# GpSimd writes the last 64 mixed columns twice; a pair of tiles leaves PSUM by one copy and one subtraction

## The reference: what is computed

```python
w = exp(weight_gen - max(weight_gen, axis=-1))       # (4, 4096, 8 heads, 7 taps)
w = w / (sum(w, axis=-1) + 1e-9)
# causal window of 7 rows, each head (24 columns) with its own weights
mix = einsum('bshk,bskhg->bshg', w, x_unfolded)       # (16384, 192)
h = mix @ w_in                                        # 192 -> 2048
g = where(h > 0, h, exp(min(h, 0)) - 1)
out = g @ w_out                                       # 2048 -> 192
```

## Time and profile before

| | |
|---|---|
| median of three runs | 1265.78 us |
| span of the profiled execution, first to last instruction | 1264.7 us |
| PE busy | 1207.9 us, 96% |
| PEld busy | 1088.5 us, 86% |
| ACT busy | 966.0 us, 76% |
| DVE busy | 822.4 us, 65% |
| POOL busy | 704.2 us, 56% |
| instruction fetches, queue 14 | 74 packets, 0.61 MB |
| instruction fetches, queue 8 | 10 packets, 0.16 MB |

### The profile page before, as it was taken

One profiled execution on the slowest core, in us unless ns is written; L12 is line 12 of the kernel. 1 busy time (PEld: TensorE's weight loads), 2 busy tenths in 40 slices (PEclk: granted clock), 3 DMA queues, 4 the chain that ended last, 5 costly groups with the idle time before them and its releaser, 6 DMA issues.

```text
span 1264.7 us, 21620 instructions
## 1 busy us (share of the span) xinstructions
PE 1207.9 (96%) x6848; PEld 1088.5 (86%) x6848; DVE 822.4 (65%) x1453; ACT 966.0 (76%) x1897; POOL 704.2 (56%) x298
## 2 busy tenths in 40 slices
PE   2799999999999999999999999999999999999998
PEld 2699998989899898998989989898998989989998
DVE  7866666666566666666666566666666666666665
ACT  3588878778788787787778787787777877877886
POOL 8666654556645466554566545566454665545600
PEclk9899999999999999999999999999999999999999
DMA  7011011111011110011110011110111100110000
GB/s 223 32 48 49 14 36 47 47 48 47 1 47 47 48 47 31 18 47 48 47 48 20 28 47 47 48 47 1 47 47 48 47 21 27 47 48 13 13 14 13
DMA packets 17124, 52.13 MB, mean 41 GB/s; under 512 B 1944, under 2 KB 8212, under 8 KB 17040
## 3 DMA queue, kind: packets, MB, share of 16 engines
q1 hardware_dynamic: 17040, 51.36, 12.0%
HBM read 38.77 MB, written 12.58 MB: 41 GB/s over the span
## 4 chain that ended last, share of the span: by engine, by line
PE 88%; issue 5%; DVE 4%; ACT 3%; DMA 0%; SPq 0%; ACTq 0%; POOL 0%; DVEq 0%; POOLq 0%
PE slot L593 44%; PE acc L599 27%; PE acc L603 15%; ACT em L425 1%; DVE wout L503 1%; PE slot L581 1%; DVE g_lo L554 1%; ACT em L431 1%; DVE slot L548 1%; ACT g_hi L438 1%; PE slot L583 1%; DVE prod L471 0%; DVE prod L475 0%; DMA xwin<-in_x_dram 0%; SPq L242 0%
## 5 line engine op out<-in xcount | busy, mean ns | idle before, releaser
L548 DVE SCALAR_TENSOR_TENSOR slot<-em,slot 128x512 f32<-128x512 f32 x512 | 356.4, 696 | 419.2 <-ACT em L431 417.6
L599 PE MATMUL acc<-wout,g_hi 128*128 128x384 f32 x2048 | 469.7, 342 | 29.0 <-DVE g_lo L554 29.0
L425 ACT ACTIVATE em<-slot 128x512 f32<-128x512 f32 x512 | 305.4, 597 | 232.7 <-PE slot L593 183.8
L599 PEld LDWEIGHTS acc<-wout,g_hi 128*128 128x128 f32 x2048 | 369.2, 188 | 71.0 <-DVE g_lo L554 26.1
L554 DVE TENSOR_TENSOR g_lo<-slot,g_hi 128x512 fp32r<-128x512 f32 x511 | 350.1, 685 | 1.9
L431 ACT ACTIVATE em<-em 128x512 f32<-128x512 f32 x512 | 323.5, 632 | 16.3
L603 PE MATMUL acc<-wout,g_lo 128*128 128x192 f32 x2048 | 327.0, 266 | 0.9 <-DVE g_lo L554 0.9
L603 PEld LDWEIGHTS acc<-wout,g_lo 128*128 128x128 f32 x2048 | 312.0, 190 | 3.2 <-DVE g_lo L554 1.2
L331 POOL TENSOR_TENSOR prod<-xwin,probs 128x5376 f32<-128x5376 f32 (+1 forms) x32 | 308.1, 9628 | 8.1 <-POOL probs L317 6.5
L438 ACT ACTIVATE g_hi<-slot 128x512 fp32r<-128x512 f32 x511 | 298.1, 583 | 12.8 <-DVE slot L548 11.3
L593 PE MATMUL slot<-xt,win_hi 128*128 128x512 f32 x512 | 214.9, 420 | 2.7 <-DVE xt L516 2.7
(11 more groups left out here) (47 smaller groups left out, 585.1 us busy)
## 6 DMA issues: line engine op xcount, KB each, us to landing
xwin<-in_x_dram SPq DMA_DIRECT2D x30, 960.0 KB, 4.7
out_dram<-outs SPq DMA_DIRECT2D x32, 384.0 KB, 2.4
wg<-in_weight_gen_dram SPq DMA_DIRECT2D x32, 112.0 KB, 2.3
wout_raw<-in_moe_w_out_dram SPq DMA_DIRECT2D x4, 384.0 KB, 9.5
win_raw<-in_moe_w_in_dram SPq DMA_DIRECT2D x1, 768.0 KB, 6.5
win_rest_raw<-in_moe_w_in_dram SPq DMA_DIRECT2D x2, 384.0 KB, 8.6
xwin<-in_x_dram SPq DMA_DIRECT2D x1, 768.0 KB, 11.0
xwin<-in_x_dram SPq DMA_DIRECT2D x1, 384.0 KB, 3.7
```

Of the source, the lines that this page charges most:

```text
L425: nc.scalar.activation(em[:, i % 2, :], slot[s][:], ACT.Exp).then_inc(s_exp, 1)
L548: nc.vector.scalar_tensor_tensor(out=slot[s][:], in0=em[:, i % 2, :], scalar=0.0, in1=slot[s][:], op0=ALU.min, op1=ALU.max).then_inc(s_g, 1)
L599: pe.matmul(acc[j][:, 0:2 * d_model], g_hi[:, f % GBUFS, chunk(j)], wout[:, f, :], start=(f == 0), stop=False)
```

## The change

GpSimd (and VectorE in the first block) writes each tile's last 64 columns twice side by side, so `mixed_rest` has 128 columns for each tile. TensorE transposes each tile's rest by itself, two transposes where there was one, and the slot is filled with 512 columns; both halves of the partitions hold the same 64 columns. ScalarE copies the whole slot at once to hi, and VectorE makes lo of it by one subtraction. The split of the weights moves into one array: `win_rest` has hi of w_in's last 64 rows on partitions 0 to 63 and lo on 64 to 127, so the subtraction that makes lo runs on 64 partitions. The five matmuls of the first product stay five: the two for the rest are now (hi; lo) of the weights with hi of x, and (hi; lo) with lo of x.

```diff
--- before.py
+++ after.py
@@ -72,7 +72,7 @@
-    XPARTS = 3
+    XPARTS = 1
@@ -121,8 +121,7 @@
-        win_rest_hi = sb("win_rest_hi", [P, d_ff], F32R)
-        win_rest_lo = sb("win_rest_lo", [P, d_ff], F32R)
+        win_rest = sb("win_rest", [P, d_ff], F32R)
@@ -135,10 +134,10 @@
-        mixed_rest = sb("mixed_rest", [P, 2, TILES, REST])
+        mixed_rest = sb("mixed_rest", [P, 2, TILES, 2, REST])
...
-        xt_lo = sb("xt_lo", [P, 2, N], F32R)
+        xt_lo = sb("xt_lo", [P, 2, 2, N], F32R)
@@ -224,6 +223,10 @@
+        def twice(t, tiles):
+
+            return t[:, :, P:].unsqueeze(2).broadcast_to([P, tiles, 2, REST])
+
@@ -307,8 +310,10 @@
-                    nc.gpsimd.tensor_tensor(win_rest_lo[:, cols], win_rest_raw[:, cols],
-                                            win_rest_hi[:, cols].bitcast(F32), ALU.subtract).then_inc(s_plo, 1)
+                    pool.wait_ge(s_psoft, b.count(SOFTMAX, 1))
+                    nc.gpsimd.tensor_tensor(win_rest[REST:, cols], win_rest_raw[REST:, cols],
+                                            win_rest[REST:, cols].bitcast(F32), ALU.subtract).then_inc(s_plo, 1)
+                    pool.wait_ge(s_plo, 1)
@@ -345,8 +350,8 @@
-                nc.gpsimd.tensor_tensor(mixed_rest[:, q, first_tile:, :], one[:, :, P:], two[:, :, P:],
-                                        ALU.add).then_inc(s_add, 1)
+                nc.gpsimd.tensor_tensor(mixed_rest[:, q, first_tile:, :, :], twice(one, TILES - first_tile),
+                                        twice(two, TILES - first_tile), ALU.add).then_inc(s_add, 1)
@@ -383,16 +388,13 @@
-                nc.scalar.activation(xt[:, parity, 0, k * W:(k + 1) * W], slot[s][:, 0:W], ACT.Copy).then_inc(s_xhi, 1)
-                for t in range(PAIR):
-                    half_of = slice(t * REST, (t + 1) * REST)
-                    nc.scalar.activation(xt[half_of, parity, 1, k * W + t * P:k * W + (t + 1) * P],
-                                         slot[s][half_of, W:W + P], ACT.Copy).then_inc(s_xhi, 1)
+                nc.scalar.activation(xt[:, parity, :, k * W:(k + 1) * W],
+                                     slot[s][:].rearrange("p (a c) -> p a c", a=2), ACT.Copy).then_inc(s_xhi, 1)
...
-                parts = ((win_hi, win_raw), (win_rest_hi, win_rest_raw))
+                parts = ((win_hi, win_raw), (win_rest, win_rest_raw))
@@ -484,7 +486,7 @@
-                    nc.vector.tensor_tensor(mixed_rest[:, q, 0:tiles, :], one_t[:, :, P:], two_t[:, :, P:],
+                    nc.vector.tensor_tensor(mixed_rest[:, q, 0:tiles, :, :], twice(one_t, tiles), twice(two_t, tiles),
@@ -492,10 +494,12 @@
-            for k, (lo, raw, hi) in enumerate(((win_lo, win_raw, win_hi), (win_rest_lo, win_rest_raw, win_rest_hi))):
-                dve.wait_ge(s_whi, 1 + k)
-                nc.vector.tensor_tensor(lo[:, cols], raw[:, cols], hi[:, cols].bitcast(F32),
-                                        ALU.subtract).then_inc(s_wlo, 1)
+            dve.wait_ge(s_whi, 1)
+            nc.vector.tensor_tensor(win_lo[:, cols], win_raw[:, cols], win_hi[:, cols].bitcast(F32),
+                                    ALU.subtract).then_inc(s_wlo, 1)
+            dve.wait_ge(s_whi, 2)
+            nc.vector.tensor_tensor(win_rest[REST:, cols], win_rest_raw[REST:, cols],
+                                    win_rest[REST:, cols].bitcast(F32), ALU.subtract).then_inc(s_wlo, 1)
@@ -507,15 +511,8 @@
-                nc.vector.tensor_tensor(xt_lo[:, parity, cols], slot[s][:, 0:W], xt[:, parity, 0, cols].bitcast(F32),
-                                        ALU.subtract).then_inc(s_xlo, 1)
-
-                for t in range(PAIR):
-                    half_of, other = (slice(a * REST, (a + 1) * REST) for a in (t, 1 - t))
-                    cols = slice(k * W + t * P, k * W + (t + 1) * P)
-                    nc.vector.tensor_tensor(xt[other, parity, 1, cols], slot[s][half_of, W:W + P],
-                                            xt[half_of, parity, 1, cols].bitcast(F32),
-                                            ALU.subtract).then_inc(s_xlo, 1)
+                nc.vector.tensor_tensor(xt_lo[:, parity, :, cols], slot[s][:].rearrange("p (a c) -> p a c", a=2),
+                                        xt[:, parity, :, cols].bitcast(F32), ALU.subtract).then_inc(s_xlo, 1)
@@ -579,8 +576,9 @@
-                rest = mixed_rest[:, parity, k * PAIR:(k + 1) * PAIR, :].rearrange("p t c -> p (t c)")
-                last = pe.transpose(slot[s][:, W:W + P], rest, ident[:])
+                for t in range(PAIR):
+                    rest = mixed_rest[:, parity, k * PAIR + t, :, :].rearrange("p a c -> p (a c)")
+                    last = pe.transpose(slot[s][:, W + t * P:W + (t + 1) * P], rest, ident[:])
@@ -588,8 +586,8 @@
-                        (win_hi[:, cols], xt_lo[:, parity, :]), (win_rest_hi[:, cols], xt[:, parity, 1, :]),
-                        (win_rest_lo[:, cols], xt[:, parity, 1, :]))):
+                        (win_hi[:, cols], xt_lo[:, parity, 0, :]), (win_rest[:, cols], xt[:, parity, 1, :]),
+                        (win_rest[:, cols], xt_lo[:, parity, 1, :]))):
```

## The result

The changed kernel takes 1247.99 us (median of 4 runs, 1247.65 to 1248.53), before 1265.85 us. The ratio is 0.986, with a 95% interval from 0.9836 to 0.9884.

A forecast was written before the change was run, and what follows sets the result against it. TensorE, busy 1207.9 of 1264.7 us, was taken as the bound, with waits behind ScalarE's loop branch. 1265.8 + 7.1 (transposes) + 0 - 20.5 (waits gone) = 1252.4 us, range 1250 to 1257.

The forecast's parts named there:

- The branch: At ScalarE's loop branch: missing instructions delay g_lo for TensorE; the shorter program removes all 13 waits, -20.5 us.
- the pieces: ScalarE's program is fetched 128 instructions at a time; its loop needs four such parts in place of five.
- the second silence: ScalarE's 2.04 us stop right behind the loop's first instruction; it goes whether three or four pieces are held.
- Which of three or four pieces is held: ScalarE's instruction memory: with four nothing is fetched in the loop; with three one stop of 1.96 us remains.
- The rival that the silences stay: ScalarE still fetches two pieces in a row at each of 13 branches; transposes cost alone, 1272.9 us; chance 0.12.
- the other rule of size: Trainium skill's window, two blocks of 256 instructions: a loop over a border fetches at every branch, before and after.
- the 13 waits of the list: TensorE's waits for g_lo behind the branch, 1.58 us each, 20.5 us together, all expected to go.
- The transposes: On TensorE, one more for each pair, 62 outside the fill, up to 0.115 us each: +7.1 us.
- Copies, subtractions, GpSimd in the loop: ScalarE and VectorE together 0.64 us less for each pair, GpSimd's mixed_rest 0.6 to 0.7 us longer but hidden: 0.
- The start: The fill: longer mixed_rest and two added transposes against a shorter copy and subtraction chain, -0.6 to +0.9 us, taken as 0.
- One silence left: Behind ScalarE's branch: one stop of 2.9 us outlasts TensorE's slack, 13 x 0.5 = 6.5 us, so 1259; chance 0.05.
- its own branch: TensorE's loop branch, no longer hidden by a wait, costs up to 0.3 us: +3.9, so 1256; chance 0.05.

The follow-up runs named there:

- the second trace: The unchanged kernel before, run once more for its trace: 1264.58 us.
- The experiment with one instruction: The kernel before with one spare semaphore increment ahead of ScalarE's program, nothing else changed: 1242.48 us, ratio 0.9811.
- The kernel with the transposes alone: The kernel before plus one spare ScalarE instruction, with each pair's third transpose made twice, three copies and subtractions kept: 1250.33 us.
- The kernel with three transposes: The changed kernel, from block 1 on without the transpose of the second tile's rest (output partly wrong): 1241.59 us.
- the experiment with one silence: The changed kernel with 5 spare instructions ahead of ScalarE's loop and 17 in it: 1248.20 us, ratio 0.9851.
- the kernel with the splits at chunks 6, 10 and 14: The kernel before plus one spare ScalarE instruction, with w_out's last three splits moved from chunks 1, 2, 4 of block 0: 1245.67 us.
- the one kernel whose waits there were 2.1 and 1.0 us: The kernel before plus one spare ScalarE instruction, with w_out's splits at chunks 0, 0, 11, 12 of block 0: 1234.96 us, ratio 0.9742.

## Why the prediction was right or wrong

**The branch: the mechanism right, the term too small.** The term that decided was what the pieces do, and each step of it held: where the loop begins, how many pieces it needs, that the second silence is the one that costs. Which of three or four pieces is held, open in the prediction, is settled at four. The rival that the silences stay has fallen, and so has the other rule of size. The Trainium skill ("Runtime: NRT & Kernel Launch", section "Instruction fetch mechanics") has blocks of 256 instructions, two of them held; with the loop over a border in both kernels there would be no gain. The traces say 128 and four for ScalarE, with the loop at five placements (instructions ahead of it and in it): 189 and 261 or 182 and 270 fetch in each turn, 177 and 253, 190 and 261, and 189 and 257 do not.

The failed step is the size of this term: the prediction took the 13 waits of the list, 29.0 - 8.5 = 20.5 us, as all that TensorE loses. A block with a branch is longer by more. Thirty blocks of the first trace, from mark to mark, 79.97 to 1227.38 us, take 1147.41 us; at 37.42 they would take 1122.6, so 24.8 us were lost. Of these 1.6 belong to the one block with the lower clock, which the second trace doesn't have. The rest is 23.2 us, 1.79 for each branch, and 1.72 in the second trace. The list counts idle time from where a matmul is modelled to end, about 0.16 us after the next could have started (0.39 us long, 0.23 from one to the next), and from the first matmul with g_hi behind the wait to the next it is 0.37 us where it is otherwise 0.28; the block that follows gets 0.05 us back (37.37 for 37.42). That makes 0.20 of the 0.21 us by which a branch costs more than its 1.58 us in the list. The experiment with one instruction measured 24 us in whole runs. Some of that may be the clock again: over the 15 runs of before that stand beside it, the time goes from 1264.09 us at a mean granted clock of 0.997 to 1270.37 us at 0.992, while the runs of the kernel with the spare instruction have 0.996 and 0.997. No trace of a run at 0.992 was kept, so this isn't shown.

**The transposes: right in kind, low in size.** I took 0.115 us each from the chain, 7.1 us in all. They cost 0.27 / 2 = 0.135 us, so 31 x 0.27 = 8.4 us; part of the difference is that the second products behind them also get a little longer. The kernel with the transposes alone shows it.

**Copies, subtractions, GpSimd in the loop: right, nothing.** The kernel with three transposes has the block of before to the hundredth.

**The start: taken as 0, was -1.4 us in the trace** (block 1's mark at 78.61 in place of 79.97). The bounds allowed -0.6. The prediction had looked at the chain up to TensorE's first product and not past it, where the larger wait is. The clock hides some of the gain: it was 0.50 for 6.8 us of the start in this trace of before, and for 10.2 us in that of the changed kernel. With 10.2 us in both it is 80.58 and 78.61, with 6.8 us in both 79.97 and, in two of the kernels with the change's start, 78.33 and 77.25. In these pairs the mark is 1.6 to 2.7 us earlier. VectorE's splits and GpSimd's product in the kernel before and the changed one, in the order of their timelines:

```profile
29.02 9.70 POOL L331 TENSOR_TENSOR prod<-xwin,probs 128x5376 f32<-128x5376 f32 x1
...
29.35 10.18 DVE L503 TENSOR_TENSOR wout<-wout_raw,wout 128x768 fp32r<-128x768 f32 x1
```

```profile
29.70 0.95 DVE L507 TENSOR_TENSOR wout<-wout_raw,wout 128x768 fp32r<-128x768 f32 x1
29.70 10.51 POOL L336 TENSOR_TENSOR prod<-xwin,probs 128x5376 f32<-128x5376 f32 x1
...
31.77 9.26 DVE L507 TENSOR_TENSOR wout<-wout_raw,wout 128x768 fp32r<-128x768 f32 x1
```

In the changed kernel VectorE's second split comes just ahead of the product, and the third is the one that is held up; between them VectorE finishes one g_lo, and TensorE has more to do meanwhile. This second split and the product start within the same hundredth, so I can't say which operation of the change gave the lead. That it is the shorter chain of copies, and not the transposes, is likely: the kernel with four transposes and three copies has its mark at 80.01 us, those of the changed kernel at 77.3 to 78.9. No run took the copies alone. The Trainium skill ("SBUF — State Buffer", section "SBUF: two separate sides") says that a VectorE operation with two SBUF inputs and a GpSimd operation that reads SBUF exclude each other for their whole length. The traces agree: the split takes 10.2 us beside a product of 9.7 and 0.9 us with none, the product takes 10.5 us where a split stands at its start, and the operations of VectorE with one input in PSUM keep their 0.68 to 0.70 us beside it.

The three sizes make up the miss: -24.8 for -20.5 (1.6 of it the clock in that one block, a chance of that trace and not the branch), +8.2 for +7.1 between the marks, -1.4 for 0, together 4.6 us; the time was 4.4 below the forecast. The range was too narrow: I had given the sure terms of the sum (the wait times, the transposes) no error of their own, and kept the width for the rivals.

**The other rivals.** One silence left did not cost TensorE anything (the experiment with one silence), and its own branch shows nowhere: blocks with and without it are equally long in the changed kernel.

## What to carry to other kernels

When an engine stands still behind a loop's branch with nothing to wait for, count its instructions and look at the fetches before anything else: a saving or a loss of 2% hung on one instruction here, and a change that shortens a program can get the credit for it. Test every such change against a kernel that differs only in the length and place of its loop. The cost of a wait is read from the period of the work, not from the list of idle times, which was 12% too low here; and an operation that excludes another engine is moved to where that engine is quiet: moved without looking at that engine, it met the next collision here. A long wait of TensorE can cost more than its own length, when the clock falls in it and the work behind it starts at the lower one (about 1.7 us more in the start here); look at the granted clock in the start, too.

## What the runs showed of the hardware

ScalarE's program is fetched in pieces of 128 instructions (8192 bytes), four are held, and a loop that needs five with the one ahead fetches all five in each turn. From the branch to the loop's first instruction it was 2.4 to 2.9 us where that piece was missing and 0.2 to 0.3 where it was held, and a second piece missing right behind it stopped ScalarE for about 2 us more (2.0 to 2.3 in the 13 turns of the first trace). TensorE's packets have 16384 bytes, and its loop of 476 instructions by the table, 904 if the weight loads of its 428 matmuls are counted apart, fetched nothing in a turn.

A VectorE subtraction with both inputs in SBUF that takes 0.9 us by itself took 10.2 us beside a GpSimd product of 9.7 us. TensorE's granted clock fell to 0.50 in or right behind the long wait of the start and stayed there for 6.8 or 10.2 us (in the kernel with the splits at chunks 6, 10 and 14 twice for 6.8); it was 1.00 all through the start in the one kernel whose waits there were 2.1 and 1.0 us.
